# Three orders of work around the split of weights, the third tile and the scatters in an attention and expert-layer kernel

## The chip, the cores and the metric

The kernel runs on one core of a Trainium2 chip. The metric is the device time of one execution, in microseconds (us). The core has five engines that run at the same time and wait for each other by semaphores: TensorE (PE in the profile: matmuls and transposes into PSUM, with its weight loads shown as PEld), VectorE (DVE), ScalarE (ACT), GpSimd (POOL) and SyncE (SP), which here only issues DMAs. Each engine works through its own list of instructions in order, so an instruction that waits holds up all that stand behind it on its engine.

## What is computed

```python
# q, k, v: (2, 8, 768, 64) -> attention with 4 sink keys and a window of 128
scores = scale * q @ k^T ; masked ; softmax ; @ v          -> x (1536, 512)
# first layer, d_ff = 2048
h = x @ w_in ; g = max(h, 0) + alpha * min(h, 0) ; x = g @ w_out
# second layer: 8 experts, d_ff = 1024, capacity 384, one expert for each token
expert_idx = argmax(x @ w_gate)
disp[e, slot] = x[token]
y = relu(disp @ w1[e]) @ w2[e]
out[token] = gate_w[token] * y[expert_idx[token], slot]
```

All is fp32. Where a matmul has more than one part of weight (the two layers, the scores), an fp32 operand is split into a high part (cast to fp32r, by ScalarE) and a low part (the fp32 value less the high part, by VectorE), and three matmuls (high x high, high x low, low x high) take the place of one.

## The kernel before

The 1536 tokens are 12 tiles of 128, and 6 chunks of two tiles. **First stage.** One list of steps n = 0 to 118 (`each_step`) is gone through by every engine, each doing its share of a step. Attention works on pairs of heads: pair p belongs to tile t = p // 4, and its scores are computed in step n = 2p. The rest of the pair follows with lags that `pair_at(n, lag)` gives: maximum and mask on VectorE and `exp` on ScalarE in the same step, the inverse of the sum (VectorE) and the normalising (GpSimd) two steps on, the transposes `p_T` and their copy `evac_p` four steps on, the product with v six steps on. `tile_at(n, lag)` does the same for tiles of 8 steps. The first three tiles are the opening (`OPENING` = 3): for tiles 1 and 2 (`early`) q and k are transposed in two parts, the first pair of heads two steps ahead of the tile (n = 6 and 14), the rest one step ahead of it, so that `qk_high(t, 0)`, the high part of that first pair on ScalarE, and then `q_low`, `k_low` on VectorE stand in step 14 for the third tile (t = 2). In the opening, TensorE has little to do and runs transposes of the identity that nobody reads (`keep_busy(k, bank)`, k of them).

From step 22 on (`OPEN` = 22) the first layer runs beside it: in step n = 23 + m TensorE computes `hidden(m + 1)`, one block of 128 hidden columns for a chunk of 256 tokens (12 matmuls), and then `y_sum(m)`, what block m adds to the output of the chunk (6 matmuls, 128x512). Between them stand VectorE L1518, L1523 (the activation), ScalarE L844 (its high part) and VectorE L1529 (its low part). A chunk has 16 blocks.

The weights of the first layer are 32 pieces of 128x512: 16 of `w_in` and 16 of `w_out`, in the order in which the blocks of the first chunk want them. A piece is loaded by SP into one of 4 slots, split by ScalarE (`weights_high`, L710) and then VectorE (`weights_low`, L1316), and stays. How many are split by the end of step n is `split_by(n)`: seven up to step 21, then one in each step, and one more in odd steps and in those of a hand-written set. A piece is split at the end of its step's work on VectorE, and SP loads into the slot when it is free. For the first chunk `y_sum(m)` waits for 6 + 2m pieces (17 + m from m = 11 on), and `hidden` for 4, 11, 19 and 27 pieces at m + 1 = 0, 4, 8, 12.

**Second stage.** The outputs go to memory, the router picks an expert, and the tokens of each expert are gathered by GpSimd into slot tiles (3 for each of the 8 experts: item 3e + j; the second and third are skipped, by a branch on the count of tokens, where an expert has too few). `X_ORDER` has the first tile of the next expert ahead of the second and third of this one. For expert e the order on TensorE is `expert_in` (24 matmuls), the transposes of x for the next expert, `expert_out` of the last tile of the expert before (24 matmuls), `hidden_T`, then in pairs for the second and third tiles. ScalarE has the relu, the high parts of the next tiles' x, the first 8 of 16 pieces of the next expert's weights, `scaled` (L893: the last output of the expert before, times the gate, into one of two buffers `o_sb`), `hidden_high`, the other 8 pieces with a relu between them, and again `scaled`. `scaled(i)` waits until the scatter of item i - 2 has landed, which frees its buffer. A skipped tile's semaphores are raised by marks (`Busy.mark`, and the last argument of `scaled`). GpSimd issues, for each item i in turn, one gather (`gather_to`, L647, item number 9 + i in `X_ORDER`) and then the scatter of item i (L662). Weights come through 11 slots on SP's queue, gathers and scatters through GpSimd's.

Of the kernel before, what the change touches and what calls it, by code (L numbers as in the profile page):

```python
# [15 lines left out]
def sparse_attention_then_two_expert_layers(  # L16
# [40 lines left out]
    TPC = 2  # L57
# [26 lines left out]
    with ctx:  # L84
# [305 lines left out]
        def split_by(n):  # L390

            early = sum(k > 2 and k % 2 == 0 and k % H != 0 for k in range(min(n + 1, OPEN)))
            late = sum(1 + (k % 2 == 1 or k in (OPEN, OPEN + 6)) for k in range(OPEN, n + 1))
            return min(early + late, NP1)

        def v_of(t):
# [178 lines left out]
        def _(pool):  # L575
# [78 lines left out]
            def gather_to(last):  # L654
                for i in gathers:
                    gather(i)
                    if i >= last:
                        break
# [14 lines left out]
            last = NA - TPE  # L673
            for i in range(last):

                gather_to(i + 8)
                scatter(i)
            gather_to(NA)
            busy = Busy(pool)
            busy.load((E - 1,))  # L680
# [24 lines left out]
        def _(act):  # L705
# [105 lines left out]
            def step(c, i, n):  # L811
                t = tile_at(n, H + 5)
                if t is not None:
                    tile_end(t)
                t = tile_at(n, -1)
                if t is not None:
                    qk_high(t, 1 if early(t) else 0)
                moved = pair_at(n, 4)
                if n > OPEN and moved is not None:
                    evac_p(moved)  # L820
                if n < OPEN:
                    for p in range(split_by(n - 1), split_by(n)):
                        weights_high(p)
                p = pair_at(n, 0)
                if p is not None:
                    exp(p)
                t = tile_at(n, -2)
                if t is not None and early(t):
                    qk_high(t, 0)
                if n <= OPEN and moved is not None:  # L830
                    evac_p(moved)
                t = tile_at(n, H + 3)
                if t is not None and has_sinks(t):
                    if t % QT == 2:
                        v_sink_high(t // QT)
                    sink_prob_high(t)
                if c >= 1 and i in (0, 2):
                    evac_yT(TPC * (c - 1) + i // 2)
                m = NF * c + i + 1
                if 0 <= m < NF * NC:  # L840
                    act.wait_ge(activation_done, m + 1)
                    if m >= 2:
                        act.wait_ge(y_done, m - 1)
                    act.copy(g_hl[m % 2][:, 0, :], g_full[:, m % 2, :]).then_inc(activation_high_split, 1)  # L844
                if n >= OPEN:
                    for p in range(split_by(n - 1), split_by(n)):
                        weights_high(p)
                if c >= 1 and i == 4:
                    router_exp(c - 1)
                if c == NC - 1 and i == NF - 1:  # L850
                    some(0, 2, 0)
                if c >= 0 and i == NF - 1:
                    y_out(c)
# [52 lines left out]
            for e in range(E):  # L906
# [10 lines left out]
                else:  # L917
# [3 lines left out]
                    second_tile(e)  # L921
                    with act.Else():
                        busy.mark(expert_relu_done, 4)
                    some(0, W1, e + 1)
                    busy.last_of(e - 1, scaled)
                    split = W1
                hidden_high(first)
                with busy.over(e, 1):
# [26 lines left out]
        def _(pe):  # L955
# [174 lines left out]

            keep_busy(10, Y_BANK[1])
            first_pair_T(first_q_loaded, O_BANK, q_raw)
            keep_busy(1, Y_BANK[1])
            first_pair_T(first_k_loaded, P_BANK, k_raw)
            q_T(0)
            k_T(0)
            keep_busy(3, Y_BANK[1])

            def step(c, i, n):
                m = NF * c + i  # L1140
# [512 lines left out]
```

## Time and profile before the change

| | |
|---|---|
| time, median of 3 runs | 626.91 us (622.16 to 627.31) |
| profiled execution | 624.89 us, span 623.1 us |
| busy: TensorE, its weight loads | 594.3 us (95%), 505.2 us (81%) |
| busy: VectorE, ScalarE, GpSimd | 354.5 us (57%), 282.3 us (45%), 141.6 us (23%) |
| mean granted clock of TensorE | 0.985 |
| chain that ended last | TensorE 89%, VectorE 4%, ScalarE 2%, DMA 1% |

The span is from the first to the last instruction of one execution, taken with the profiler; the execution's own time is the figure to set beside the runs. "Busy" is the time in which an engine has an instruction under way, and matmuls overlap. A granted clock of 1.00 is 2.4 GHz, 0.50 is 1.2 GHz. "Idle before" is the time that an engine stood still ahead of an instruction, and the releaser is what ended it; "issue" means that the profile shows no releaser. Releasers are inferred, and where an engine waits for several things, the last one is named.

### The profile page before, as it was taken

The numbers are of one execution on the slowest core, as the hardware profiler recorded it, in microseconds if no ns is written. First come the engines' busy times: TensorE is split into PE (matmuls) and PEld (weight loads), VectorE is DVE, ScalarE is ACT, GpSimd is POOL, SyncE is SP. The second block draws the span as 40 slices with busy tenths as digits, with TensorE's granted clock in tenths as the row PEclk, the third lists the DMA queues.
The fourth block names the chain that finished last, engine by engine and source line by source line (L and its number), as shares of the span: only waits on it lengthen the run. The fifth ranks groups of instructions, "written<-read, shape, count | busy, mean of one in ns | idle before, by whom it ended". The sixth has DMA issues, their size and how long they took to land.

```text
span 623.1 us, 11538 instructions
## 1 busy us (share of the span) xinstructions
PE 594.3 (95%) x3904; PEld 505.2 (81%) x3904; DVE 354.5 (57%) x1035; ACT 282.3 (45%) x681; POOL 141.6 (23%) x188
## 2 busy tenths in 40 slices
PE   8899968999999999999999999998999999899994
PEld 7678856888888888888888889978788888688883
DVE  5778854565455645565556445546744487389300
ACT  5766632533243334433433221123745496489421
POOL 5312221212211222222222200003302152235101
PEclk9999998999999999999999999998999999899998
DMA  7435440201041502010100050006863779299100
GB/s 187 127 102 144 132 127 17 70 18 36 19 131 47 140 22 70 2 32 21 53 1 18 1 203 1 1 33 194 282 236 86 289 222 366 101 362 358 42 19 19
DMA packets 73271, 67.45 MB, mean 108 GB/s; under 512 B 42884, under 2 KB 49044, under 8 KB 73200
## 3 DMA queue, kind: packets, MB, share of 16 engines
q1 hardware_dynamic: 68464, 57.50, 29.0%
q0 software_dynamic: 3680, 8.77, 4.6%
q8 instruction: 41, 0.67, 0.4%
q10 hardware_dynamic: 1056, 0.26, 0.2%
q14 instruction: 30, 0.25, 0.1%
HBM read 57.75 MB, written 12.06 MB: 112 GB/s over the span
## 4 chain that ended last, share of the span: by engine, by line
PE 89%; DVE 4%; issue 2%; ACT 2%; DMA 1%; POOL 0%; SPq 0%; DVEq 0%; POOLq 0%; ACTq 0%
PE bank L967 23%; PE bank L969 22%; PE bank L968 22%; PE bank L957 11%; PE bank L1039 4%; PE bank L1011 4%; PE bank L1107 1%; DVE wl L1316 1%; DMA fw<-y_scratch,mask 1%; DVE fw L1518 1%; DVE rw L1337 1%; DMA o_sb<-in_q_dram 1%; DVE fw L1523 1%; PE bank L1054 1%; ACT wh L710 0%
## 5 line engine op out<-in xcount | busy, mean ns | idle before, releaser
L967 PE MATMUL bank<-wh,rw 128*128 128x512 f32 x416 | 168.2, 404 | 12.5 <-DVE wl L1316 8.4
L969 PE MATMUL bank<-wh,rw 128*128 128x512 f32 x416 | 164.1, 395 | 0.0
L968 PE MATMUL bank<-wl,rw 128*128 128x512 f32 x416 | 163.8, 394 | 0.0
L967 PE MATMUL bank<-rw,wh 128*128 128x256 f32 x384 | 113.5, 296 | 0.0
L969 PE MATMUL bank<-rw,wl 128*128 128x256 f32 x384 | 109.0, 284 | 0.0
L968 PE MATMUL bank<-rw,wh 128*128 128x256 f32 x384 | 108.8, 283 | 0.0
L844 ACT CAST rw<-fw 128x256 fp32r<-128x256 f32 x96 | 39.0, 406 | 145.0 <-DVE fw L1523 144.7
L967 PEld LDWEIGHTS bank<-wh,rw 128*128 128x128 f32 x416 | 78.8, 190 | 27.3 <-DVE rw L1529 10.5
L969 PEld LDWEIGHTS bank<-wh,rw 128*128 128x128 f32 x416 | 78.7, 189 | 17.2
L628 POOL TENSOR_SCALAR fw<-fw,rinv 128x256 f32<-128x256 f32 (+1 forms) x88 | 75.6, 870 | 64.3 <-DVE rinv L1371 64.2
L968 PEld LDWEIGHTS bank<-wl,rw 128*128 128x128 f32 x416 | 78.9, 190 | 12.6
L1316 DVE TENSOR_TENSOR wl<-fw,wh 128x512 fp32r<-128x512 f32 x127 | 81.3, 687 | 10.0 <-ACT wh L710 8.6
L1518 DVE TENSOR_SCALAR fw<-bank,alpha_sb 128x256 f32<-128x256 f32 x96 | 46.4, 483 | 70.6 <-PE bank L969 70.5
L967 PEld LDWEIGHTS bank<-rw,wh 128*128 128x128 f32 x384 | 73.1, 190 | 2.7 <-DVE rw L1394 0.2
L710 ACT CAST wh<-fw 128x512 fp32r<-128x512 f32 x127 | 71.9, 623 | 6.0 <-DMA fw<-in_moe_w_dram 4.2
L968 PEld LDWEIGHTS bank<-rw,wh 128*128 128x128 f32 x384 | 73.1, 190 | 1.6
L969 PEld LDWEIGHTS bank<-rw,wl 128*128 128x128 f32 x384 | 73.1, 190 | 0.0
L1529 DVE TENSOR_TENSOR rw<-fw,rw 128x256 fp32r<-128x256 f32 x96 | 41.2, 430 | 43.0 <-ACT rw L844 43.0
L957 PE MATMUL bank<-ident,fw 128*128 128x128 f32 x392 | 60.9, 282 | 2.9 <-DMA fw<-y_scratch,mask 1.2
L757 ACT COPY fw<-bank 128x512 f32<-128x512 f32 (+1 forms) x48 | 26.3, 549 | 65.5 <-PE bank L957 65.4
L957 PEld LDWEIGHTS bank<-ident,fw 128*128 128x128 f32 x392 | 43.6, 141 | 14.3 <-issue 3.6
L623 POOL TENSOR_TENSOR fw<-fw,rinv 128x24 f32<-128x24 f32 x32 | 7.4, 231 | 195.5 <-DVE rinv L1371 195.5
(121 smaller groups left out, 681.7 us busy)
## 6 DMA issues: line engine op xcount, KB each, us to landing
fw<-in_moe_w_dram SPq DMA_DIRECT2D x95, 256.0 KB, 5.7
v_raw<-in_moe_w_dram SPq DMA_DIRECT2D x22, 256.0 KB, 5.9
fw<-in_moe_w_in_dram SPq DMA_DIRECT2D x16, 256.0 KB, 3.2
fw<-in_moe_w_out_dram SPq DMA_DIRECT2D x16, 256.0 KB, 2.7
y_scratch<-fw SPq DMA_DIRECT2D x12, 256.0 KB, 2.0
out_dram<-v_or_route SPq DMA_DIRECT2D x12, 256.0 KB, 3.5
v_raw<-in_v_dram SPq DMA_DIRECT2D x11, 256.0 KB, 2.9
o_sb<-in_q_dram SPq DMA_DIRECT2D x11, 256.0 KB, 3.3
```

The costliest lines, as they stand in the source:

```text
L628: pool.tensor_scalar(x, x, rinv[:, 2 * r + a:2 * r + a + 1], None, ALU.mult).then_inc(prob_normalised, 1)
L710: act.copy(wh[:, hf, col:col + PIECE], staged).then_inc(weights_high_split, 1)
L757: act.copy(pT[:, cs], P_BANK[:, cs]).then_inc(probT_evacuated, 1)
L844: act.copy(g_hl[m % 2][:, 0, :], g_full[:, m % 2, :]).then_inc(activation_high_split, 1)
L957: return pe.transpose(dst, src, ident[:, :])
L967: pe.matmul(dst, ah, bh, start=start, stop=False, skip_group_check=True)
L968: pe.matmul(dst, ah, bl, start=False, stop=False, skip_group_check=True)
L969: return pe.matmul(dst, al, bh, start=False, stop=stop, skip_group_check=True)
L1011: m = pe.matmul(S_BANK[a][:, 0:width(t)], x[ds, :], y[ds, 0:width(t)], start=i == 0, stop=i == 2)
L1316: dve.tensor_tensor(wl[:, hf, col:col + PIECE], staged, f32(wh[:, hf, col:col + PIECE]), ALU.subtract).then_inc(weights_low_split, 1)
L1518: dve.tensor_scalar(g_neg[:, :], hb, 0.0, alpha_sb[:, m % NF:m % NF + 1], ALU.min, ALU.mult).then_inc(negative_part_done, 1)
L1529: dve.tensor_tensor(g_hl[m % 2][:, 1, :], g_full[:, m % 2, :], f32(g_hl[m % 2][:, 0, :]), ALU.subtract).then_inc(activation_low_split, 1)
```

## The change

There are five edits. (1) In `split_by`, the set of even steps with one piece more becomes 22, 26 and 30 in place of 22 and 28. (2) GpSimd issues the scatter ahead of the gather for the items with i % 3 == 1. (3) On ScalarE, `qk_high(t, 0)` of the third tile stands ahead of `exp` in step 14 (the second tile's stays behind), and in step 22 `evac_p` stands ahead of `exp` as in later steps. (4) In the expert stage ScalarE's `scaled` of the expert before stands behind six of the next expert's first eight pieces, and two pieces behind it. (5) In TensorE's prologue the four spare transposes after the first ten are spread differently: two after the first pair of q and two after that of k, ahead of `q_T(0)`, and none before the first scores.

```diff
--- before.py
+++ after.py
@@ -390,7 +390,7 @@
         def split_by(n):
 
             early = sum(k > 2 and k % 2 == 0 and k % H != 0 for k in range(min(n + 1, OPEN)))
-            late = sum(1 + (k % 2 == 1 or k in (OPEN, OPEN + 6)) for k in range(OPEN, n + 1))
+            late = sum(1 + (k % 2 == 1 or k in (OPEN, OPEN + 4, OPEN + 8)) for k in range(OPEN, n + 1))
             return min(early + late, NP1)
 
         def v_of(t):
@@ -673,8 +673,11 @@
             last = NA - TPE
             for i in range(last):
 
+                if i % TPE == 1:
+                    scatter(i)
                 gather_to(i + 8)
-                scatter(i)
+                if i % TPE != 1:
+                    scatter(i)
             gather_to(NA)
             busy = Busy(pool)
             busy.load((E - 1,))
@@ -816,18 +819,20 @@
                 if t is not None:
                     qk_high(t, 1 if early(t) else 0)
                 moved = pair_at(n, 4)
-                if n > OPEN and moved is not None:
+                if n >= OPEN and moved is not None:
                     evac_p(moved)
                 if n < OPEN:
                     for p in range(split_by(n - 1), split_by(n)):
                         weights_high(p)
+                t = tile_at(n, -2)
+                if t is not None and early(t) and t >= TPC:
+                    qk_high(t, 0)
                 p = pair_at(n, 0)
                 if p is not None:
                     exp(p)
-                t = tile_at(n, -2)
-                if t is not None and early(t):
+                if t is not None and early(t) and t < TPC:
                     qk_high(t, 0)
-                if n <= OPEN and moved is not None:
+                if n < OPEN and moved is not None:
                     evac_p(moved)
                 t = tile_at(n, H + 3)
                 if t is not None and has_sinks(t):
@@ -921,8 +926,9 @@
                     second_tile(e)
                     with act.Else():
                         busy.mark(expert_relu_done, 4)
-                    some(0, W1, e + 1)
+                    some(0, W1 - 2, e + 1)
                     busy.last_of(e - 1, scaled)
+                    some(W1 - 2, W1, e + 1)
                     split = W1
                 hidden_high(first)
                 with busy.over(e, 1):
@@ -1130,11 +1136,11 @@
 
             keep_busy(10, Y_BANK[1])
             first_pair_T(first_q_loaded, O_BANK, q_raw)
-            keep_busy(1, Y_BANK[1])
+            keep_busy(2, Y_BANK[1])
             first_pair_T(first_k_loaded, P_BANK, k_raw)
+            keep_busy(2, Y_BANK[1])
             q_T(0)
             k_T(0)
-            keep_busy(3, Y_BANK[1])
 
             def step(c, i, n):
                 m = NF * c + i
```

## Rows read from the trace of the kernel before

**Rows 1.** Page, costliest groups: busy us, mean ns | idle before it, releaser

```profile
L967 PE MATMUL bank<-wh,rw 128*128 128x512 f32 x416 | 168.2, 404 | 12.5 <-DVE wl L1316 8.4
```

**Rows 2.** Windows: length, busy us of each engine, PEclk, DMA share, GB/s

```profile
5.00:37.00 32.00, 30.10 (x265) 23.46 (x266) 22.14 (x95) 22.88 (x73) 12.63 (x23) 1.00 0.61 163
37.00:80.00 43.00, 42.07 (x312) 35.90 (x311) 35.82 (x94) 26.82 (x66) 10.54 (x16) 1.00 0.43 126
80.00:104.00 24.00, 15.57 (x94) 12.39 (x93) 10.05 (x28) 6.60 (x17) 2.68 (x5) 0.86 0.28 72
92.40:95.20 2.80, 2.80 (x14) 2.64 (x12) 0.29 (x1) 0.26 (x1) 0.00 (x0) 0.51 0.20 73
100.00:102.00 2.00, 2.00 (x15) 1.44 (x14) 0.00 (x0) 0.00 (x0) 0.00 (x0) 0.50 0.00 0
532.80:536.00 3.20, 3.20 (x8) 2.53 (x9) 1.29 (x2) 1.06 (x2) 0.00 (x0) 0.50 0.15 49
```

**Rows 3.** Timeline, steps 32 to 35: start, us, instruction [idle before <-releaser]

```profile
79.71 0.69 DVE L1316 TENSOR_TENSOR wl<-fw,wh 128x512 fp32r<-128x512 f32 x1
...
80.27 0.28 PE L969 MATMUL bank<-rw,wl 128*128 128x256 f32 x1
...
83.36 0.47 PE L967 MATMUL bank<-wh,rw 128*128 128x512 f32 x1 [2.81 <-DVE wl L1316]
...
98.17 0.47 PE L967 MATMUL bank<-wh,rw 128*128 128x512 f32 x1 [2.81 <-DVE wl L1316]
```

**Rows 4.** Timeline of TensorE, step 25

```profile
49.14 0.50 PE L967 MATMUL bank<-wh,rw 128*128 128x512 f32 x1 [0.27 <-DVE rw L1529]
```

**Rows 5.** Timeline, steps 14 to 18

```profile
25.95 0.24 ACT L722 CAST rw<-bank 128x128 fp32r<-128x128 f32 x1
...
26.23 0.29 DVE L1337 TENSOR_TENSOR rw<-bank,rw 128x128 fp32r<-128x128 f32 x1 [0.96 <-ACT rw L722]
...
26.82 0.62 PE L1011 MATMUL bank<-rw 64*128 64x260 f32 x6 [1.21 <-DVE rw L1337]
...
29.63 0.63 PE L1011 MATMUL bank<-rw 64*128 64x260 f32 x6 [0.47 <-issue]
```

**Rows 6.** Timeline, prologue and first steps

```profile
6.38 0.85 PE L957 MATMUL bank<-ident 128*128 128x128 f32 x3
...
7.16 0.55 PE L1011 MATMUL bank<-rw 64*128 64x128 f32 x6
...
8.38 0.55 DVE L1347 TENSOR_TENSOR rw<-bank,rw 128x384 fp32r<-128x384 f32 x1
...
9.03 0.55 PE L1011 MATMUL bank<-rw 64*128 64x128 f32 x6 [0.18 <-issue]
```

**Rows 7.** Timeline of TensorE, expert stage

```profile
528.78 1.03 PE L957 MATMUL bank<-ident,fw 128*128 128x128 f32 x8
...
532.76 0.76 PE L967 MATMUL bank<-wh,rw 128*128 128x512 f32 x1 [2.94 <-issue]
```

**Rows 8.** Timeline of ScalarE, expert stage

```profile
516.64 1.25 ACT L710 CAST wh<-fw 128x512 fp32r<-128x512 f32 x2 [0.54 <-DMA fw<-in_moe_w_dram]
...
519.29 1.16 ACT L710 CAST wh<-fw 128x512 fp32r<-128x512 f32 x2 [1.40 <-DMA fw<-in_moe_w_dram]
...
520.35 0.68 ACT L893 ACTIVATE o_sb<-bank,inv 128x512 f32<-128x512 f32 x1
...
531.94 0.69 ACT L893 ACTIVATE o_sb<-bank,inv 128x512 f32<-128x512 f32 x1 [4.55 <-DMA out_dram<-o_sb,mask]
```

**Rows 9.** Timeline of GpSimd, expert stage

```profile
521.86 1.02 POOL L662 DMA_INDIRECT out_dram<-o_sb,mask  x1 [8.66 <-ACT o_sb L893]
...
523.19 1.44 POOL L647 DMA_INDIRECT fw<-y_scratch,mask  x1 [0.31 <-issue]
...
524.93 1.50 POOL L662 DMA_INDIRECT out_dram<-o_sb,mask  x1 [0.30 <-issue]
```

**Rows 10.** All scatters of L662, from issue to landing

```profile
DMA to landing us min/median/max: 2.2/5.2/7.2
```

## The prediction

> **What bounds the kernel now.** The table of busy times in the page comes first: TensorE is busy for 594 of 623 us, so nearly everything is decided by what makes TensorE wait or run slowly, and the gain of any edit is the TensorE time that it frees. The page's groups give the largest such item: matmuls of L967 sat idle for 8.4 us until a VectorE L1316, the low part of a piece of weights, had ended [rows 1]. The windows then say where: between 80 and 104 us TensorE is busy for only 15.6 of 24 us and its mean granted clock is 0.86, while between 37 and 80 us it is busy for 42 of 43 us at 1.00 [rows 2]. The timeline shows the wait itself, 2.81 us three times, in steps 33, 34 and 35 (the starts 83.36 and 98.17 are the first and the third) [rows 3]. A second, smaller hole lies at 529.8: 2.94 us of TensorE idle, after which 3.2 us run at a granted clock of 0.50 [rows 2, 7]. Elsewhere from 104 to 615 us it hardly waits, so a gain made early is carried to the end.
>
> **Part 1, the split_by table.** `split_by(n)` says how many pieces are split by the end of step n. Before it gives 24, 25, 27, 28, 30 for n = 31 to 35; after it gives 25, 26, 28, 29, 31. `y_sum(m)` runs in step 23+m and needs 6+2m pieces up to m = 11, then 17+m: 26 in step 33, 28 in step 34, 29 in step 35. Before, each of these is split only in the very step that needs it, behind VectorE's and ScalarE's work on the hidden block that TensorE has just finished, so TensorE stands still. After, each is split one step earlier. The three waits are 3 x 2.81 = 8.4 us. Behind the second one the granted clock falls to 0.51 and 0.50, the lower of the two levels, 1.2 GHz [rows 2]; the stage was idle 2.8 us twice within 11 us before this. Lost there: 2.8 x 0.49 + 2.0 x 0.50 = 2.4 us from the two short windows, and at most 24 x 0.14 = 3.4 us from the whole one. I take 2.9.
>
> What it costs: nothing is added, one VectorE subtraction (0.69 us; a start every 0.60 in a run of them) and one ScalarE copy are moved from step 28 to 26 and from 37 to 30. So from step 30 on VectorE is 0.6 us later than before. VectorE has no reserve here: it is busy 35.8 of 43 us, and the rest is its fixed wait for ScalarE in each step [rows 2]; one y_sum already waited 0.27 us for it [rows 4]. The 26th piece, split at 79.71 to 80.40, therefore ends at about 81.0, while the last matmul before y_sum(10) starts at 80.27 and y_sum could start at 80.4 [rows 3]. With 0.12 us for the semaphore it starts at 81.1 instead of 83.36: of the first 2.81 us, 0.6 stay. In the next two steps TensorE has 4.6 us and 3.1 us of work between two y_sums, VectorE needs about 3.2 us in each, and I find both pieces ready 0.4 to 1.5 us ahead. Part 1: 8.4 + 2.9 - 0.6 = **10.7 us**. Its loads move with it: SP fills a slot when the piece four before is split, so loads are issued earlier, never later.
>
> **Part 2, step 14 and step 22.** Before, ScalarE splits the third tile's first pair after `exp(7)`: it begins at 25.95, VectorE's low parts follow at 26.23 after 0.96 us idle, and the scores of step 16 start at 26.82 after 1.21 us in which TensorE had nothing [rows 5]. ScalarE would have been free for it before, since the transposes end at 24.2 and it waits for VectorE's maximum anyway. After, the split is hidden in that wait, VectorE goes on at about 25.3, and these scores start at about 25.9: 0.9 us. VectorE then has its usual queue, so the scores of step 18 (29.63 [rows 5]) come 0.7 us earlier. I take 0.7. In step 22 `evac_p(9)` passes `exp(11)`; it frees 0.66 us of TensorE before the transposes of step 23, but VectorE is the later one two steps on [rows 4], so I count 0 (up to 0.6).
>
> **Part 3, the prologue.** The three spare transposes before the first scores go; they take 6.38 to 7.16, while their inputs had been ready [rows 6]. Against that three more stand ahead of q_T(0), which waited 0.2 us for its load; so k's first pair is one transpose (0.21 us) later and q_T(0) 0.2 us later. Net: scores(0) at about 6.7 instead of 7.16, 0.45 us. scores(1) at 9.03 follows a VectorE k_low of 8.38 to 8.93 [rows 6], which stands behind the first maxima, so it moves too. I take 0.4, between 0 and 0.5. Parts 2 and 3 reach hidden(0) through work that is in one chain: **1.1 us**.
>
> **Part 4, the expert stage.** The hole at 529.8 has no releaser in the profile ("issue"). By the code `expert_in(12)` waits for `expert_relu_done`, which ScalarE marks for the absent third tile behind `scaled(9)`; and `scaled(9)` sat idle 4.55 us until a scatter had landed, and ran 531.94 to 532.63; TensorE went on at 532.76 [rows 7, 8]. The scatter it needs is that of slot tile 7, issued at 524.93, behind a gather of 523.19, behind the scatter of tile 6 at 521.86, which waited for `scaled(6)`, done at 520.35 behind the last two of eight pieces, themselves late by a load (1.40 us) [rows 8, 9]. Both edits shorten just this chain. Six pieces end at 517.9 [rows 8], `expert_out(6)` at 517.2, so `scaled(6)` goes 2.4 us earlier; and 7 % 3 == 1, so scatter(7) passes the gather (1.7 us: 523.19 to 524.93). It is issued at about 520.8 and lands, with the same 7.0 us from issue (524.93 to 531.9 [rows 8, 9]; the longest seen is 7.2 [rows 10]), at 527.8. `scaled(9)` then waits only for `expert_out(9)`, which ends at 528.9, and TensorE goes on at about 529.9. Gain 2.9 us, and 3.2 x 0.50 = 1.6 us of clock [rows 2]: **4.5 us**. With either edit alone it would land at 529.5 to 530.2 and a hole of up to 1.2 us would stay.
>
> The Trainium skill ("DMA: Bandwidth & Descriptors", section "Anatomy of one DMA") gives about 2.0 us plus the bytes over 436 GB/s for such a transfer, 2.6 us for 256 KB as an estimate. By that scatter(7) would have landed at 527.5 before the change already, there would be no hole, and part 4 would be worth nothing; the trace disagrees (median 5.2 us, up to 7.2 [rows 10]), with the engines full of weights at that time, and the trace decides.
>
> What these edits put at risk: where `expert_out` of the expert before ends after six pieces, ScalarE stands idle ahead of two pieces that it could have split. In experts 1, 2 and 4 this puts it back by up to two pieces, 1.05 us, and behind it `hidden_high`, the next relu, `x_high` and the pieces, VectorE's counterparts, and then SP's loads of the slots. Their users come 3 to 5 us later, so I count 0. The gathers that are now behind a scatter fetch tiles used an expert or more later: 0.
>
> **Sum.** 10.7 + 1.1 + 4.5 = 16.3 us. Of the profiled execution's 624.9 us 608.6 stay. That execution is 2.0 us below the median of the three runs (626.9), and I don't know whether this spread outlives the waits; I add a small part of it and say 609.
>
> **Rivals.** (a) *The scatter stays late*, since its landing depends on the weights in the DMA engines, or another ScalarE wait takes the hole's place: part 4 is lost, 613.1. For it: such transfers took from 2.2 to 7.2 us [rows 10]. Against: 1.1 us of margin. (b) *VectorE becomes the bound in the first chunk*: 0.6 us of extra lag at a place without reserve could leave half of each wait and the clock with it: 5.3 us less, 613.9. For it: rows 4 and the busy share; against: VectorE sat idle in steps 33 to 35 only because TensorE did. (c) *The pieces are not the cause*: y_sum also needs the low part of the activation (L1529), and if that had been the last, the waits would shrink by the pieces' 0.8 us only: 2.4 us for part 1, 616.9. Against: y_sum(10)'s activation was split in step 32. (d) *The other side, slower*: with the three spare transposes gone, TensorE loses its clock in the opening. Its 30.1 busy us from 5 to 37 us would at half clock cost up to 30 us [rows 2]: 624.9 - 15.2 + 30 = 640. It decides once more than 15.2 us are lost. The Trainium skill ("TensorE: Matmul & The Clock Gate", Part 1) says that the throttled state is the default and activity releases it, which speaks against taking spare work out; against it here, the same number of transposes is moved earlier rather than removed (three out, three in), and the granted clock was 1.00 throughout.
>
> **How the numbers follow.** Forecast 0.60 (own range 606 to 612), (a) 0.15, (b) 0.12, (c) 0.05, (d) 0.03; 0.05 is left for more gain than I count (step 22's 0.6, the 0.6 of lag). The range reaches from 605 to 616, over (a) and (b) with the runs' spread of 2 us. A measurement of this kernel can tell about 1%, 6.3 us, from no change: faster means under 620.6. All cases but (d) lie there; with a margin for what I have not seen, 0.94 faster, 0.04 within 1%, 0.02 slower.
>
> **What would show it.** L967's wait for L1316 falls from 8.4 us to about 0.6, and the clock between 80 and 104 us stays at 1.00; scores of step 16 without the 1.2 us wait; no 2.9 us hole after the eighth expert transposes, and ScalarE's `scaled(9)` waiting for TensorE, not a DMA. I am wrong if the waits are found again on L1529 or L1359, if `scaled` still waits for a scatter, or if the clock falls in a place where it was 1.00.

## The result and the profile after

Changed: 609.38 us, median of 6 runs (607.86 to 610.74). Before, on the same chip: 626.46 us, median of 6 runs (620.06 to 627.31). The ratio is 0.9751, 95% interval 0.9705 to 0.9797: faster by 2.5%. The profiled execution took 607.86 us with a span of 606.1, against 624.89 and 623.1 before: 17.0 us less, where the prediction's sum said 16.3.

The diff moves the lines of the kernel: L967, L1316 and L1529 of before are L973, L1322 and L1535 after; ScalarE's L710 and L893 are L713 and L898; each experiment has small shifts of its own. First the group of the page that answers to [rows 1]:

```profile
L973 PE MATMUL bank<-wh,rw 128*128 128x512 f32 x416 | 167.1, 402 | 2.2 <-DVE rw L1535 1.3
```

And TensorE's waits (who waited, line, for whom: us in total, times, longest):

```profile
PE bank L963 <- POOL ident L584: 1.6, 1, 1.6
PE bank L973 <- DVE rw L1535: 1.3, 2, 0.8
...
PE bank L973 <- DVE wl L1322: 0.5, 1, 0.5
PE bank L973 <- issue: 0.3, 1, 0.3
```

The idle time ahead of this group fell from 12.5 to 2.2 us, and what was 8.4 us behind the low part of a piece of weights is 0.5. The 1.3 us behind L1535 (0.8 before) are the waits of two y_sums for the activation; the one of [rows 4] grew from 0.27 to 0.76. The windows, with the columns of [rows 2], say the same of the stretch:

```profile
5.00:37.00 32.00, 31.22 (x279) 24.66 (x278) 23.25 (x100) 24.78 (x79) 13.76 (x24) 1.00 0.60 162
37.00:80.00 43.00, 41.45 (x305) 35.24 (x303) 36.35 (x92) 25.64 (x63) 9.41 (x14) 1.00 0.48 142
80.00:104.00 24.00, 23.75 (x178) 20.19 (x177) 16.45 (x48) 12.97 (x33) 6.09 (x9) 1.00 0.24 68
...
515.00:520.00 5.00, 5.00 (x27) 4.07 (x26) 1.29 (x2) 1.76 (x3) 1.83 (x2) 1.00 0.93 351
520.00:597.00 77.00, 76.94 (x379) 64.35 (x378) 40.17 (x65) 44.59 (x83) 22.29 (x19) 1.00 0.47 166
```

From 80 to 104 us TensorE is busy for 23.75 of 24 us (15.57 before), at a granted clock of 1.00 (0.86 before). VectorE has 36.35 busy us between 37 and 80 instead of 35.82, in a window that now holds slightly later work, since hidden(0) comes 1.7 us earlier. The timeline of TensorE shows the three places of [rows 3], now y_sum(10), (11) and (12):

```profile
78.43 0.29 PE L975 MATMUL bank<-rw,wl 128*128 128x256 f32 x1
79.22 0.47 PE L973 MATMUL bank<-wh,rw 128*128 128x512 f32 x1 [0.50 <-DVE wl L1322]
...
83.85 0.39 PE L973 MATMUL bank<-wh,rw 128*128 128x512 f32 x1
...
86.83 0.47 PE L973 MATMUL bank<-wh,rw 128*128 128x512 f32 x1
```

Two of the waits are gone and 0.50 us of the first stays. Where the 17.0 us went, by four marks on TensorE's timeline (start of the first matmul of each):

| stretch | before, us | after, us | difference |
| --- | --- | --- | --- |
| start to hidden(0) | 36.66 | 34.99 | -1.67 |
| hidden(0) to the last y_sum | 379.94 | 368.58 | -11.36 |
| last y_sum to the wait for the first slot gather (router) | 17.27 | 17.88 | +0.6 |
| that wait to the end (experts) | 189.2 | 184.6 | -4.6 |

The third row is not the edits' doing. In the fourteen profiled executions of this study that stretch takes 17.25 to 19.83 us with no order by kernel; the changed kernel itself took 17.88 in this execution and 19.52 in another. It ends with a wait of 0.6 to 3.0 us for the gather, and TensorE's granted clock in it differs from execution to execution: 0.90 in that of before, 0.81 in that of the changed kernel, 1.00 in one of the kernels below. So two executions of one kernel can differ here by up to 2.6 us, and the two of the table are nearer to each other than that by chance.

### The profile page after: what moved, and what is told of

It is laid out like the page before. It is cut to its first block, busy times and chain, and to the rows that moved or that the text cites. A ratio compares the mean times of both kernels' runs of the same rounds, so it can differ in the third digit from the quotient of the medians.

```text
span 606.1 us, 11538 instructions
## 1 busy us (share of the span) xinstructions
PE 589.9 (97%) x3904; PEld 503.3 (83%) x3904; DVE 353.3 (58%) x1035; ACT 282.5 (47%) x681; POOL 143.1 (24%) x188
## 4 chain that ended last, share of the span: by engine, by line
PE 86%; DVE 6%; issue 3%; ACT 3%; DMA 1%; POOL 0%; DVEq 0%; POOLq 0%; ACTq 0%
PE bank L973 22%; PE bank L975 21%; PE bank L974 21%; PE bank L963 12%; PE bank L1045 4%; PE bank L1017 4%; PE bank L1113 2%; DVE wl L1322 1%; DVE fw L1524 1%; DVE fw L1529 1%; ACT wh L713 1%; DMA fw<-y_scratch,mask 1%; DVE fw L1365 1%; DVE rw L1343 1%; ACT rw L849 1%
## 5 line engine op out<-in xcount | busy, mean ns | idle before, releaser
L973 PE MATMUL bank<-wh,rw 128*128 128x512 f32 x416 | 167.1, 402 | 2.2 <-DVE rw L1535 1.3
L973 PE MATMUL bank<-rw,wh 128*128 128x256 f32 x384 | 112.7, 294 | 0.0
L975 PEld LDWEIGHTS bank<-wh,rw 128*128 128x128 f32 x416 | 78.1, 188 | 17.1
L973 PEld LDWEIGHTS bank<-wh,rw 128*128 128x128 f32 x416 | 78.3, 188 | 16.2 <-DVE rw L1535 2.6
L1322 DVE TENSOR_TENSOR wl<-fw,wh 128x512 fp32r<-128x512 f32 x127 | 81.0, 687 | 9.2 <-ACT wh L713 6.5
L973 PEld LDWEIGHTS bank<-rw,wh 128*128 128x128 f32 x384 | 72.5, 189 | 2.7 <-DVE rw L1400 0.2
L713 ACT CAST wh<-fw 128x512 fp32r<-128x512 f32 x127 | 72.0, 623 | 2.8 <-DMA fw<-in_moe_w_dram 1.6
L1535 DVE TENSOR_TENSOR rw<-fw,rw 128x256 fp32r<-128x256 f32 x96 | 41.5, 432 | 43.0 <-ACT rw L849 43.0
L963 PEld LDWEIGHTS bank<-ident,fw 128*128 128x128 f32 x392 | 43.3, 140 | 14.1 <-issue 3.3
L647 POOL DMA_INDIRECT fw<-y_scratch,mask x20 | 24.5, 1225 | 116.7 <-DVE mask L1569 79.0
```

The costliest lines, as they stand in the source:

```text
L647: pool.indirect_dma_start(out=x_slot[k % GR], out_offset=None, in_=y_dram, in_offset=bass.IndirectOffsetOnAxis(ap=gid[:, 0, i:i + 1], axis=0),
L713: act.copy(wh[:, hf, col:col + PIECE], staged).then_inc(weights_high_split, 1)
L963: return pe.transpose(dst, src, ident[:, :])
L973: pe.matmul(dst, ah, bh, start=start, stop=False, skip_group_check=True)
L975: return pe.matmul(dst, al, bh, start=False, stop=stop, skip_group_check=True)
L1322: dve.tensor_tensor(wl[:, hf, col:col + PIECE], staged, f32(wh[:, hf, col:col + PIECE]), ALU.subtract).then_inc(weights_low_split, 1)
```

## The experiments

The runs e1 to e4 share a chip (before: 626.03 us, median of 7), e5 to e8 another (624.80, median of 11), e9 to e12 a third (623.67, median of 11). Edits are numbered as in the section on the change.

### One part alone: the table

Kernel before plus edit 1:

```diff
-            late = sum(1 + (k % 2 == 1 or k in (OPEN, OPEN + 6)) for k in range(OPEN, n + 1))
+            late = sum(1 + (k % 2 == 1 or k in (OPEN, OPEN + 4, OPEN + 8)) for k in range(OPEN, n + 1))
```

> The kernel before with edit 1 alone, the table of split_by. My theory (the three waits of 2.8 us and the clock lost behind them come from pieces that are split in the step that needs them): the waits of the first 128x512 matmul of y_sum(10), (11), (12) go from 2.81, 2.81, 2.81 us to about 0.5, 0, 0, the granted clock between 80 and 104 us is 1.00, and about 10.7 us go, 626 to 615. The hole of 2.9 us in the expert stage stays. Rival (the low part of the activation is what comes last): the waits shrink to about 2 us each and are put down to VectorE's low part of the activation; about 2.4 us go. Rival (VectorE becomes the bound): waits of about 1.4 us are left at each place, 5 us go.

> The kernel before with edit 1 alone, once more. Theory A: 1 to 3 us slower than the changed kernel, of which 1.05 us are the split of step 14 (the scores of step 16 follow those of step 14 after 4.25 us here and after 3.2 us with the edit, in every execution). Theory B: 5 to 6 us slower. The prologue: unedited ones had their first scores at 6.25 to 7.16 us, edited ones at 6.54 and 6.83, so I expect 6.2 to 7.2 again here and no difference by the edit.

Measured: 609.96 us (4 runs), ratio 0.9755 [0.9694, 0.9816], and on the second chip 612.97 (6 runs, 609.37 to 615.96), ratio 0.9816 [0.9781, 0.9851]. Both profiled executions have a span of 609.8. The wait at y_sum(10) is what was expected, 0.45 us in the first and 0.55 in the second; y_sum(11) and (12) don't wait, and the granted clock between 80 and 104 us is 1.00 in both:

```profile
81.94 0.47 PE L967 MATMUL bank<-wh,rw 128*128 128x512 f32 x1 [0.55 <-DVE wl L1316]
```

From hidden(0) to the last y_sum both take 368.5 us. So this single expression carries 11.4 of the 17.0 us between the two profiled executions, and 11.8 to 16.1 us by medians. The first median with its four runs looked as good as the whole change; with six runs, and the changed kernel timed on the same chip, it was 4.3 us behind it (between the two expectations, 1 to 3 and 5 to 6), so only the second is fit to divide the gain. The hole of the expert stage, expected to stay at 2.9 us, was 1.49 us in the first execution and absent in the second; the section on undoing the expert edits takes that up.

### The waits without the clock

Kernel before, with eleven spare transposes ahead of the wait for the pieces in each of the three steps, so that TensorE stands still for 1.5 us instead of 2.8 three times, and nothing else changes:

```diff
                     pe.wait_ge(activation_low_split, m + 1)
+                    if m in (10, 11, 12):
+                        for _ in range(11):
+                            tr(H_BANK[m % 2][:, 3 * P:4 * P], ident[:, :])
```

> The kernel before, with 11 spare transposes on TensorE in each of the steps 33, 34 and 35, between the wait for the low part of the activation and the wait for the pieces. They fill most of each wait with work that nobody reads. Theory: the waits themselves stay, since the pieces come no earlier (y_sum(10) starts at about 83.4 in both), but the granted clock stays 1.00 from 92 to 103 us and about 2.9 us go, which is the share of the clock in part 1. Rival (the clock was lost for another reason): it falls to 0.5 near 92 us all the same and nothing is gained. If the transposes were more than the wait, y_sum would start later than before.

Measured: 620.65 us (1 run), span 618.9. TensorE's timeline at the three waits:

```profile
82.82 0.51 PE L967 MATMUL bank<-wh,rw 128*128 128x512 f32 x1 [1.52 <-DVE wl L1319]
...
87.48 1.36 PE L957 MATMUL bank<-ident 128*128 128x128 f32 x11
90.36 0.50 PE L967 MATMUL bank<-wh,rw 128*128 128x512 f32 x1 [1.52 <-DVE wl L1319]
...
96.28 0.50 PE L967 MATMUL bank<-wh,rw 128*128 128x512 f32 x1 [1.52 <-DVE wl L1319]
```

And the window of the stretch, columns as in [rows 2]:

```profile
80.00:104.00 24.00, 19.45 (x146) 16.45 (x145) 11.45 (x31) 8.64 (x22) 4.05 (x6) 1.00 0.26 68
```

The wait for L1319 (this kernel's L1316) is the pieces' low part, and it ends no earlier than before: y_sum(10) starts 46.58 us after hidden(0), against 46.70. The idle time is merely shorter because the transposes fill it, 1.3 us each time. What changes is the granted clock, 1.00 through the whole window in place of 0.86, and the stretch from hidden(0) to the last y_sum takes 377.04 instead of 379.94 us: 2.9 us for the clock alone. The other 8.5 us (377.04 - 368.55) are the waits. This divides part 1 for the profiled execution of before, which its own profile could not do: 8.5 of waiting, 2.9 of clock. It rests on one execution of this kernel, but on a stretch that repeats closely where the clock stays at 1.00.

### The other parts alone

Kernel before plus edits 2 and 4 (experts only), and kernel before plus edits 3 and 5 (opening only):

```diff
+                if i % TPE == 1:
+                    scatter(i)
...
-                    some(0, W1, e + 1)
+                    some(0, W1 - 2, e + 1)
                     busy.last_of(e - 1, scaled)
+                    some(W1 - 2, W1, e + 1)
```

> The kernel before with edits 2 and 4 (scatter ahead of the gather for i % 3 == 1, and scaled behind six of eight pieces). Theory: the hole of 2.94 us at 529.8 and the half clock behind it go, 4.5 us in all; scaled(9) waits for TensorE and for no DMA. The first chunk's three waits of 2.81 us stay. Rival (the scatter stays late, as its landing hangs on the weights in the DMA engines): a hole of 1 us or more is left.

> The kernel before with edits 3 and 5 (the third tile's split ahead of exp, evac_p in step 22, the prologue). Theory: the scores of step 2 start 0.6 us earlier, those of step 16 1.7 us earlier than in the kernel before, hidden(0) 1.7 us earlier. Since VectorE is without a break from hidden(0) to step 32, y_sum(10) starts 1.7 us earlier too, and its wait of 2.8 us stays. About 1.7 us go in all. Rival (the gain ends at a wait of the first chunk): y_sum(10) starts at 83.4 as before. Rival (the clock falls in the opening): granted clock below 1.00 before 37 us, slower.

Measured: 623.17 us and 623.03 us (1 run each), spans 621.4 and 621.2. Neither is more than 0.5% from the median of before: without edit 1 the rest hardly shows. All three waits of 2.81 us stay in both; in the one with edits 2 and 4 the clock behind them fell further, as the window shows:

```profile
80.00:106.00 26.00, 17.70 (x89) 13.92 (x90) 9.55 (x27) 6.54 (x16) 2.44 (x5) 0.74 0.22 59
```

hidden(0) to the last y_sum took 382.64 us here, and 378.66 with the opening's edits. Take 377.04, the value with the clock held, as the base: the same three waits cost 2.9, 5.6 and 1.6 us of clock in three executions (before, experts only, opening only). The experts' edits don't touch this stretch. Edit 3 does at its very start: with `evac_p` ahead of `exp` in step 22, y_sum(0) starts 3.85 us behind hidden(0) instead of 4.68, but y_sum(2) then waits 0.76 us for VectorE instead of 0.27 and starts 12.47 us behind hidden(0) instead of 12.48. So the difference between the three is the spread of the clock's answer.

The experts alone took 184.65 us from the wait for the first gather to the end, 4.55 less than in the profiled execution of before, with no hole and `scaled(9)` waiting for TensorE, as expected; the clock in the first stage took most of it back. With the opening's edits alone hidden(0) came at 35.60 us, 1.06 earlier than before, where 1.7 were expected.

In the opening, step 14 is told by the time from scores(7) to scores(8), which are those of steps 14 and 16. Before (starts 22.57 and 26.82, the wait of [rows 5]) they lie 4.25 us apart; the timeline of the changed kernel has:

```profile
24.57 0.28 DVE L1343 TENSOR_TENSOR rw<-bank,rw 128x128 fp32r<-128x128 f32 x1
...
25.15 0.62 PE L1017 MATMUL bank<-rw 64*128 64x260 f32 x6 [0.15 <-issue]
```

VectorE's low part starts at 24.57 instead of 26.23 and the scores at 25.15 instead of 26.82, 3.19 us behind scores(7) (21.96). The low part stands at the same place in VectorE's queue in both, directly behind the two maxima; it only waits for ScalarE no more. With edit 3 this distance is 3.19 or 3.20 in nine executions of eight kernels, without it 4.24 or 4.25 in five of five: 1.05 us, the most certain number of this study. hidden(0) has all of it: it starts 9.83 to 9.85 us behind scores(8) in all fourteen executions.

The prologue (edit 5) can't be told from the start of scores(0) alone. It is 7.16 before and 6.54 after, but the other four executions without the edit gave 6.25, 6.74, 6.53 and 7.87, and the other eight with it 6.83, 6.68, 6.07, 6.03, 6.45, 6.69, 6.69 and 5.97. Two things move it. One is the load of q, as in this execution of the table alone, whose q_T(0) waited 0.92 us where before's waited 0.21:

```profile
5.54 1.76 PE L957 MATMUL bank<-ident,o_sb 128*128 128x128 f32 x7 [0.92 <-DMA o_sb<-in_q_dram]
7.09 0.85 PE L957 MATMUL bank<-ident 128*128 128x128 f32 x3
7.87 0.90 PE L1011 MATMUL bank<-rw 64*128 64x128 f32 x6
```

The other is larger: the spacing of the transposes falls from about 0.21 to about 0.12 us at some moment, and that moment differs between executions. In the other execution of the table alone q_T(0) waited 0.16 us, hardly less than before's, yet the same seven transposes were through by 5.83 where before's took until 6.38:

```profile
4.79 1.20 PE L957 MATMUL bank<-ident,o_sb 128*128 128x128 f32 x7 [0.16 <-DMA o_sb<-in_q_dram]
5.83 0.49 PE L957 MATMUL bank<-ident 128*128 128x128 f32 x3
6.25 0.55 PE L1011 MATMUL bank<-rw 64*128 64x128 f32 x6
```

The windows print a granted clock of 1.00 there, but in the traces the records of the clock begin only at that moment, between 4.4 and 9.1 us; ahead of it the 1.00 says nothing. Executions with like moments can be compared: clock held 6.74 (records from 6.40) and changed 6.54 (6.32); before 7.16 (7.10) and the scatter made late 6.69 (7.06); experts only 6.53 (5.57) and scatter order undone 6.45 (5.73). That puts the edit at 0.1 to 0.5 us. It is no more because three spare transposes go and three come: 23 transposes stand ahead of scores(0) in both, and only TensorE's wait for q can be filled.

### Undoing the expert edits

The changed kernel as it is, with edits 2 and 4 undone, with 2 alone undone, and with 4 alone undone:

```diff
-                if i % TPE == 1:
-                    scatter(i)
                 gather_to(i + 8)
-                if i % TPE != 1:
-                    scatter(i)
+                scatter(i)
...
-                    some(0, W1 - 2, e + 1)
+                    some(0, W1, e + 1)
                     busy.last_of(e - 1, scaled)
-                    some(W1 - 2, W1, e + 1)
```

> The changed kernel as it is, timed beside the next three on the same chip. By my sum it is 17 us faster than the kernel before (626 to 609). The question of this group: edit 1 alone gave 610.0, only 0.6 us more than all five, where my sum had 5.6 us for the others. Theory A (the others are worth little, since the hole in the expert stage was 0.6 to 1.5 us in most executions and not 2.9): this one is 1 to 3 us faster than edit 1 alone. Theory B (my sum: the others are worth 5.6 us and that run was a chance): it is 5 to 6 us faster.

> The changed kernel with edits 2 and 4 undone (the scatters and scaled as before). Theory A: a hole of 0.5 to 3 us is back at expert_in(12), with the clock mostly kept; 0.5 to 3 us slower than the changed kernel. Theory B: a hole of 2.9 us and the half clock behind it, 4.5 us slower.

> The changed kernel with edit 2 alone undone (every gather ahead of its scatter). Times are told from the moment T at which TensorE has ended expert_out(9) and scaled(9) could start. With the edit scatter(7) is issued 8.3 us ahead of T, without edits 2 and 4 it was 4.1 to 6.6 us ahead, and it landed 5.3 to 7.0 us after its issue. Theory: here scaled(6) stays 11.4 us ahead of T, scatter(7) is issued about 6.9 us ahead, so the hole at expert_in(12) is 0 to 0.1 us: edit 4 alone is enough in nearly all executions. Rival (edit 2 is what counts): a hole of 0.5 us or more.

> The changed kernel with edit 4 alone undone (scaled behind all eight pieces). Theory: scaled(6) is again 8.7 to 11.2 us ahead of T, as the last two pieces' loads come late or not, and scatter(7) is issued 1.6 us behind scatter(6) instead of 3.1, so 5.6 to 8.0 us ahead of T: a hole of 0 to 1.4 us, differing from execution to execution. Rival (edit 4 is what counts): scaled(6) late and a hole of 1.5 us or more as before.

Measured: as it is 608.68 us (5 runs), ratio 0.9739 [0.9712, 0.9766]; both undone 610.98 (6 runs), 0.9799 [0.9768, 0.9829]; scatter order undone 608.71 (4 runs), 0.9736 [0.9689, 0.9784]; ScalarE's order undone 609.33 (4 runs), 0.9757 [0.9709, 0.9805]. The two edits together are worth 2.3 us by medians, and the intervals of the first two just fail to touch; either one alone can't be told from both. With both undone a hole of at least 0.5 us had been expected, and the profiled execution has none.

### A scatter made late

The changed kernel, with 16 fills on GpSimd ahead of the scatter of slot tile 7:

```diff
                 if i % TPE == 1:
+                    if i == 7:
+                        for _ in range(16):
+                            made(pool.memset(tri[:, :], 0.0))
                     scatter(i)
```

> The changed kernel with about 4.5 us of spare GpSimd work (16 fills of a table no longer used) ahead of scatter(7) alone. Theory (TensorE's hole at expert_in(12) is the landing of scatter(7), passed on by scaled(9)): scatter(7) is issued about 3.8 us ahead of T, lands 1.5 to 3.2 us behind T, scaled(9) waits for a DMA and TensorE has a hole of that size, where the changed kernel has none. Rival (the hole has another cause, such as a branch or the fetch of instructions): no hole, as in the changed kernel.

Measured: 614.09 us (1 run), span 612.4. GpSimd's, ScalarE's and TensorE's timelines:

```profile
509.57 4.16 POOL L679 MEMSET tri<- 128x128 f32 x16
514.56 1.44 POOL L662 DMA_INDIRECT out_dram<-o_sb,mask  x1 [0.83 <-POOL tri L679]
...
521.22 0.69 ACT L901 ACTIVATE o_sb<-bank,inv 128x512 f32<-128x512 f32 x1 [6.38 <-DMA out_dram<-o_sb,mask]
...
516.91 1.03 PE L966 MATMUL bank<-ident,fw 128*128 128x128 f32 x8
522.04 0.47 PE L976 MATMUL bank<-wh,rw 128*128 128x512 f32 x1 [4.09 <-issue]
```

The hole is back, with the same releasers as in [rows 7, 8]: a scatter 6.3 us behind that of tile 6 (508.27) instead of 1.6 makes `scaled(9)` wait for its landing and TensorE wait without a named releaser. That is the chain that the prediction read from the code, now made on purpose.

The table puts all of them on one line. Call lead the time from the issue of scatter(7) to the moment when `expert_out(9)` is ready for `scaled(9)` (0.19 us after the start of the eight transposes); the hole should be the landing time less the lead, and nothing where that is negative:

| kernel | edits 2, 4 | lead, us | landing, us | landing - lead | hole read | transposes to end, us |
| --- | --- | --- | --- | --- | --- | --- |
| before | none | 4.0 | 7.0 | 3.0 | 2.94 | 94.3 |
| table alone | none | 4.8 | 6.4 | 1.5 | 1.49 | 91.5 |
| clock held | none | 4.7 | 5.3 | 0.7 | 0.62 | 91.0 |
| opening alone | none | 5.2 | 6.4 | 1.2 | 1.18 | 91.2 |
| both undone | none | 6.6 | 5.8 | -0.8 | 0 | 90.4 |
| table alone, again | none | 6.3 | 5.8 | -0.5 | 0 | 90.1 |
| scatter order undone | 4 | 6.7 | 5.3 | -1.5 | 0 | 90.6 |
| ScalarE's order undone | 2 | 7.8 | 5.4 | -2.4 | 0 | 89.8 |
| after | 2, 4 | 8.3 | - | - | 0 | 89.7 |
| scatter made late | 2, 4 | 2.5 | 6.7 | 4.1 | 4.09 | 95.4 |

The landing is read at the start of `scaled(9)` where it was the last thing, and otherwise from the profile's own time to landing (the trace of the changed kernel has none), which is about 0.1 us shorter for the same scatter. For the one with both edits undone, a window that holds this scatter's issue alone says:

```profile
out_dram<-o_sb,mask POOLq DMA_INDIRECT x1, 5.8
```

With both edits the other executions (as it is, experts only, two and three pieces earlier) have leads of 7.7 to 8.4, landings of 5.3 to 5.7 and no hole. The lead varies more than the landing: without the edits `scaled(6)` starts from 8.6 us (before) to 11.2 us (both undone) ahead of that moment, and the scatters follow it. The transposes to the end take 90.1 to 94.3 us without the edits, mean 91.4 over six, and 89.7 to 90.0 with both, mean 89.8 over five: 1.6 us on average, 4.5 only against the profiled execution of before.

### Still earlier

The changed kernel with pieces split in steps where the opening had none, in place of the extra ones on even steps. The first takes steps 8 and 16 and keeps the extra of step 30, the second takes steps 8, 16 and 21 and keeps none:

```diff
-            early = sum(k > 2 and k % 2 == 0 and k % H != 0 for k in range(min(n + 1, OPEN)))
-            late = sum(1 + (k % 2 == 1 or k in (OPEN, OPEN + 4, OPEN + 8)) for k in range(OPEN, n + 1))
+            early = sum(k > 2 and k % 2 == 0 for k in range(min(n + 1, OPEN)))
+            late = sum(1 + (k % 2 == 1 or k == OPEN + 8) for k in range(OPEN, n + 1))
...
+            early = sum(k > 2 and k % 2 == 0 or k == OPEN - 1 for k in range(min(n + 1, OPEN)))
+            late = sum(1 + (k % 2 == 1) for k in range(OPEN, n + 1))
```

> The changed kernel with two more pieces split in the opening, where VectorE has idle time: one at the end of step 8 and of step 16, and none extra in steps 22 and 26 (only step 30 keeps its second piece). So VectorE carries one piece less from step 22 and two less from step 26 to 32. Theory (VectorE is the later one in the first chunk): y_sum(2)'s wait of 0.76 us goes to about 0.2, y_sum(10)'s wait of 0.50 to 0, and the time from hidden(0) to hidden(14) falls from 55.45 us by 0.6 to 1.2. Rival (VectorE has no reserve in the opening either): the scores of steps 10 and 18 start up to 0.6 us later and the sum is unchanged. As a whole 0 to 1.2 us faster than the changed kernel, too little to be told by times; the profile decides.

> The changed kernel with three pieces more in the opening (steps 8, 16 and 21) and no extra one in any even step from 22 on. Two pieces gave 1.0 us from hidden(0) to the last y_sum of the stage (368.5 to 367.55) and left a wait of 0.52 us at y_sum(2). Theory: VectorE is now earlier by another piece from step 22 on, the wait at y_sum(2) goes, and the stretch shortens to about 367.0; no opening step is later. Rival (the piece of step 21 delays hidden(0), since VectorE splits the second tile's x in that step): hidden(0) comes up to 0.6 us later and nothing is gained. Faster than the changed kernel by 1 to 1.5 us.

Measured: 607.83 us (5 runs), ratio 0.9732 [0.9704, 0.9760], and 606.89 (6 runs), ratio 0.9722 [0.9682, 0.9762]. TensorE's timeline of the second, at y_sum(10):

```profile
77.21 0.28 PE L975 MATMUL bank<-rw,wl 128*128 128x256 f32 x1
77.49 0.47 PE L973 MATMUL bank<-wh,rw 128*128 128x512 f32 x1
```

With three pieces the rest of the wait is gone; with two, 0.22 us of it stayed, where none was expected. The wait of y_sum(2) went from 0.76 to 0.52 us in both, where 0.2 and then nothing were expected. From hidden(0) to the last y_sum it is 367.55 and 367.44 us, 1.0 and 1.1 less than in the changed kernel, so the third piece is worth 0.1. Of this, 0.6 us is there at y_sum(2) already, which starts 11.87 us behind hidden(0) instead of 12.48. So VectorE's lack of reserve, which the prediction priced at 0.6 us, is real, and it is a matter of where the piece is placed. Both medians are the lowest of those timed beside them, but their intervals hold the changed kernel's ratio too: a gain of 0.2% is seen in the traces and not shown by the times.

## Why the prediction was right, and where it was right by luck

The forecast was 609.0 us in a range of 605 to 616; measured 609.4. The likeliest case came, and none of the rivals. By its steps:

**Part 1, forecast 10.7, measured 11.4 between the profiled executions.** The reading of the table was right: the residual wait stands at y_sum(10), 0.50 us where 0.6 was forecast, and the next two steps have none. The waits alone, less the residual, are worth 8.5, where the forecast's terms give 8.4 - 0.6 = 7.8: 0.7 us too little. The starts give 0.1 us more per wait than the idle time beside it (y_sum(10) to (11) takes 7.54 us with the clock held and 4.63 after, 2.91 us less, of which 1.52 + 1.29 are idle time and transposes). Another 0.26 us lies behind the waits, in three steps in which VectorE has fewer pieces left: y_sum(12) to (15) takes 12.72 us with the clock held and 12.46 after. The clock, forecast from three windows at 2.9, was 2.9 in the pair that isolates it. But it was 1.6 and 5.6 in two others, so the agreement says that the windows of that one execution were read rightly, not that the clock costs 2.9.

**Part 2, forecast 0.7, measured 1.05.** Everything ahead of step 14 comes 0.61 us earlier in this execution; with that taken off, the scores of step 16 came at 25.76 where about 25.9 was forecast, and VectorE's low part at 25.18 where about 25.3 was. The mis-sized step is "I take 0.7", from "VectorE then has its usual queue": the scores of step 18 stand 2.81 us behind those of step 16 in both kernels (29.63 before, 27.96 after), so nothing was eaten there and all of it passed on to hidden(0). Step 22 was counted at 0 for good reason: y_sum(0) comes 0.8 us earlier behind hidden(0), but y_sum(2) waits for VectorE 0.76 us instead of 0.27 [rows 4]. The "up to 0.6" showed only where VectorE had been relieved, in the kernels with pieces still earlier; that it is edit 3's share was not run by itself.

**Part 3, forecast 0.4, measured 0.1 to 0.5.** The difference of the two scores(0) is 0.6, but five executions without the edit spread over 1.6 us and nine with it over 0.9, with means of 6.91 and 6.44. What moves them most is the moment when the transposes' spacing falls, which the prediction did not have: it priced a transpose at 0.21 us and took the printed 1.00 for the clock. At like moments the edit gives 0.1 to 0.5 us, so the forecast lies inside, and no execution tells it more closely.

**Part 4, forecast 4.5, mis-sized.** The mechanism was right in every link: scatter(7) at 508.22, now 1.62 us behind scatter(6) instead of 3.07 [rows 9], `scaled(9)` waiting for TensorE instead of a landing, no hole:

```profile
516.55 0.69 ACT L898 ACTIVATE o_sb<-bank,inv 128x512 f32<-128x512 f32 x1 [2.75 <-PE bank L975]
...
506.60 1.31 POOL L662 DMA_INDIRECT out_dram<-o_sb,mask  x1 [5.23 <-ACT o_sb L898]
508.22 1.01 POOL L662 DMA_INDIRECT out_dram<-o_sb,mask  x1 [0.31 <-issue]
509.54 1.10 POOL L647 DMA_INDIRECT fw<-y_scratch,mask  x1 [0.30 <-issue]
```

Against the profiled execution of before, this gave 4.5 us, exactly as worked out. But that execution had the shortest lead and the longest landing of all, the one made late apart. With the same code here in five other executions the hole was 1.5, 1.2, 0.6, and twice nothing, and the window behind it kept a clock of 1.00. The step that failed is the one that took the hole of one execution as the kernel's: the average of this term is 1.6 us by the traces, 2.3 by medians. "With either edit alone a hole of up to 1.2 us would stay" was not seen; with one alone the leads are 6.7 and 7.8 us and the landings 5.3 and 5.4. With the 7.0 us of the profiled execution of before, the first of them would still have left 0.3.

The rule of the Trainium skill ("DMA: Bandwidth & Descriptors", "Anatomy of one DMA") that was weighed there, by which 2.6 us is an estimate for such a transfer, is off by a factor of two to three for the scatter of tile 7, which took 5.3 to 7.0 us wherever its landing was read. Yet its consequence, that there is no hole to remove, held in two of six executions without the edits, since their leads of 6.3 and 6.6 us covered landings of 5.8.

**The sum.** It came out because it was made and checked against the same execution: 16.3 forecast, 17.0 found in it. With typical values it is some 14 to 15: 1.05, 11.4 (10.1 to 14.1), 1.6 to 2.3, and 0.1 to 0.5 for the prologue. The medians of the two groups of runs that timed the changed kernel give 17.1 and 16.1 us. They agree within the intervals (0.9705 to 0.9797 is 12.7 to 18.5 us), but the sum of typical values lies on the low side by 1 to 3 us. The clock can account for 1.4 of that. An execution's span times what the clock lacked of 1.00 says at most what the clock cost it (mean granted clocks of 0.981 to 0.990 and 0.987 to 0.997): on the second chip 9.6 us on average over the eleven executions of before and 5.2 over the five of the changed kernel. That is 4.3 us between them, where the sum of typical values has 2.9, all of it behind the three waits. The two profiled executions, with 9.3 and 6.1, stand only 3.3 apart. In which stretch the rest of the 4.3 is lost is not shown; the router's is one where the traces show a clock below 1.00, before and after.

**The rivals.** (a) The scatter stays late: the one made late shows its price, 5.7 us of tail for 5.8 us of lost lead; 1.6 us of lost lead (ScalarE's order kept, the scatter's undone) still left no hole. (b) VectorE the bound: true for the 0.50 us that stayed at y_sum(10), and worth 1.1 us to remove together with the wait of y_sum(2), not 5.3. That y_sum(2) waits 0.49 us longer is not the table's doing: it waits 0.27 with the table alone and 0.76 with the opening's edits alone. (c) The pieces are not the cause: refuted by the table alone. (d) The clock lost in the opening: from the first record of the clock (6.3 us in the changed kernel's trace) to 37 us it is 1.00.

## What to carry to other kernels

When a producer's work is dealt out by a table of counts per step, write the counts beside the consumer's needs: a zero slack that repeats in several steps is worth more than it looks, because the clock falls behind the waits as well. A wait that depends on the time a DMA takes to land should be read in several executions before it is priced; read the lead between the issue and the need beside it, in each execution, and aim at a lead above the longest landing seen. And a piece of work added to an engine without reserve should be put where the engine idles early, not one step ahead of its use.

## What the runs showed of the hardware

The same three idle times of 2.8 us cost 1.6 to 5.6 us of clock in three executions, and filling about half of each with spare transposes made the cost vanish. The same scatter took 5.3 to 7.0 us from issue to landing in thirteen executions; the DMA engines moved 338 to 378 GB/s in the windows around the start of `scaled(9)` in four of them. At the start of the kernel the spacing of TensorE's transposes falls from about 0.21 to about 0.12 us between 4.4 and 9.1 us, at another moment in each execution, and a window ahead of that moment prints a granted clock of 1.00. Outside such places the stretches repeat closely: hidden(0) to the last y_sum took 368.50 to 368.58 us in eight executions of six kernels that share the table.
